# Seven block products for groups 2 to 4 of the last layer, and a shorter transposition of x^T between the layers

## The reference

```python
# 1: a recurrence over 768 time steps gives x, 3072 tokens of 320 channels
# 2: eight experts, x (3072 x 320), w1[e] (320 x 1024), w2[e] (1024 x 320)
for e in range(8):
    h = np.maximum(x @ w1[e], 0.0)
    out += P[:, e:e + 1] * (h @ w2[e])
# 3: the last layer, x = out, w_in (320 x 2048), w_out (2048 x 320)
h = x @ w_in
g = np.where(h > 0.0, h, np.exp(np.minimum(h, 0.0)) - 1.0)
return g @ w_out
```

## Time and profile before

| What | Value |
|---|---|
| Median of 3 runs | 2197.11 us (2195.76 to 2197.89) |
| Profiled execution, time | 2197.48 us |
| Profiled execution, span | 2195.5 us |
| TensorE matmul busy | 2166.0 us, 99% of the span |
| DVE busy | 1351.4 us, 62% |
| ScalarE busy | 809.8 us, 37% |
| GpSimd busy | 409.1 us, 19% |
| Experts' fast groups | about 667 to 1827 us |
| Last layer | 1827 to 2192 us |

### The profile page before, as it was taken

How to read it: one execution, slowest core, us unless ns; L and a number is a source line. 1 busy time by engine, 2 the same in 40 slices (tenths; PEclk the granted TensorE clock), 3 DMA queues, 4 the chain that set the end, 5 groups by cost and what they waited for, 6 DMA issues and landing times.

```text
span 2195.5 us, 35882 instructions
## 1 busy us (share of the span) xinstructions
PE 2166.0 (99%) x14692; PEld 1954.5 (89%) x14692; DVE 1351.4 (62%) x2429; ACT 809.8 (37%) x1429; POOL 409.1 (19%) x376
## 2 busy tenths in 40 slices
PE   8999999989999999999999999999999999999999
PEld 7899999878898999999999998999999998899898
DVE  6777777754457655555555555555555555666665
ACT  3433333323224333333333333333333333433333
POOL 4433333311143111111111111111111010010100
PEclk9999999999999999999999999999999999999999
DMA  6334333330101000000000000000000101000001
GB/s 102 64 59 64 65 61 60 60 91 29 47 20 46 27 1 27 27 1 27 27 1 27 27 1 27 27 1 27 27 1 27 27 1 27 1 27 27 1 16 58
DMA packets 193782, 70.51 MB, mean 32 GB/s; under 512 B 153424, under 2 KB 189776, under 8 KB 193616
## 3 DMA queue, kind: packets, MB, share of 16 engines
q1 hardware_dynamic: 193616, 68.19, 14.0%
HBM read 60.31 MB, written 7.86 MB: 31 GB/s over the span
## 4 chain that ended last, share of the span: by engine, by line
PE 97%; DVE 1%; ACT 0%; POOL 0%; issue 0%; DMA 0%; SPq 0%; ACTq 0%; DVEq 0%; POOLq 0%
PE up L1384 19%; PE up L1343 12%; PE yps L1441 9%; PE yps L1442 9%; PE yps L1443 9%; PE up L1391 7%; PE misc L1157 5%; PE yps L1360 4%; PE yps L1358 4%; PE yps L1359 4%; PE yps L1116 3%; PE up L1131 2%; PE up L1089 2%; PE up L1116 1%; PE up L1139 1%; PE misc L1150 1%
## 5 line engine op out<-in xcount | busy, mean ns | idle before, releaser
L1892 DVE SCALAR_TENSOR_TENSOR tok<-yps,prob,tok 128x320 f32<-128x320 f32 x672 | 343.1, 546 | 134.7 <-PE yps L1443 134.5
L1441 PE MATMUL yps<-w2h,hh 128*128 128x320 f32 x1344 | 414.9, 309 | 0.8 <-DVE hl L1875 0.3
L1443 PE MATMUL yps<-w2h,hl 128*128 128x320 f32 x1344 | 415.0, 309 | 0.0
L1442 PE MATMUL yps<-w2l,hh 128*128 128x320 f32 x1344 | 415.0, 309 | 0.0
L885 ACT ACTIVATE up<-up 128x512 f32<-128x512 f32 x252 | 146.7, 582 | 397.1 <-PE up L1384 395.5
L1441 PEld LDWEIGHTS yps<-w2h,hh 128*128 128x128 f32 x1344 | 252.5, 188 | 22.3 <-DVE hl L1875 2.0
L1442 PEld LDWEIGHTS yps<-w2l,hh 128*128 128x128 f32 x1344 | 252.3, 188 | 10.6
L1443 PEld LDWEIGHTS yps<-w2h,hl 128*128 128x128 f32 x1344 | 252.3, 188 | 0.0
L691 POOL TENSOR_TENSOR w1l<-w1l_raw,w1h 128x768 fp32r<-128x768 f32 x68 | 103.2, 1517 | 622.9 <-ACT w1h L796 622.9
L1875 DVE SCALAR_TENSOR_TENSOR hl<-up,hh 128x512 fp32r<-128x512 f32 x168 | 115.5, 688 | 161.3 <-ACT hh L897 161.3
L1875 DVE SCALAR_TENSOR_TENSOR hl<-hl_raw,hh 128x512 fp32r<-128x512 f32 x168 | 117.9, 702 | 147.8 <-ACT hh L897 147.8
(11 more groups left out here) (236 smaller groups left out, 4239.2 us busy)
## 6 DMA issues: line engine op xcount, KB each, us to landing
w2l_raw<-in_moe_w SPq DMA_DIRECT2D x16, 640.0 KB, 5.8
w1l_raw<-in_moe_w SPq DMA_DIRECT2D x32, 256.0 KB, 3.1
xr_raw<-x_dram SPq DMA_DIRECT2D x12, 512.0 KB, 4.0
w1l_raw<-in_moe_w SPq DMA_DIRECT2D x32, 128.0 KB, 3.9
wp<-in_w SPq DMA_DIRECT2D x24, 160.0 KB, 3.2
rp<-in_r SPq DMA_DIRECT2D x24, 160.0 KB, 3.1
vp<-in_v SPq DMA_DIRECT2D x48, 80.0 KB, 3.2
raw<-in_a SPq DMA_DIRECT2D x24, 160.0 KB, 3.7
```

Source lines behind the costliest of these rows:

```text
L1441: nc.tensor.matmul(o, hh[:, tile, c], wh, start=first, stop=False)
L1442: nc.tensor.matmul(o, hh[:, tile, c], wl, start=False, stop=False)
L1443: ins = nc.tensor.matmul(o, hl[:, tile, c], wh, start=False, stop=last)
L1892: nc.vector.scalar_tensor_tensor(out=acc, in0=yps[:, s, 0:DM], scalar=prob_of(blk * NSUB + s, e), in1=acc, op0=ALU.mult, op1=ALU.add).then ...
```

## The change

Groups 17 to 19 of the last layer are done in fast sets like the experts' (18 sets, numbered 84 to 101; the experts' are 0 to 83), with an order of their own (`second_set` on each engine). Group 16 stays plain. In a second set the odd block's down matmuls (`odd_down`) are issued within the next set, behind its fifth product; the next set's seventh and first product follow each other between the even block's two down slices. Each of the four tiles of a set goes through the exponential (`second_exp`), DVE's two operations (`elu`), the high part (`second_hi`) and the low part, which GpSimd makes (`second_lo`). Weights of the next group and the rest of the mixed tokens are made at places in the set called "first" and "middle" (`second_tasks`). The mixed tokens need raw rows of x^T, which ScalarE copies out of the transposes' bank (`raw_copy`). In group 16, ScalarE makes the mixed tokens of blocks 0 to 3 at steps 5 to 8, 12 to 14 and 18, and splits group 17's weights at the steps `WEIGHTS_AT`.

The tail rows of x^T are transposed once, into 64 rows; high and low part both come from these. Block 1 is transposed in the experts' last three sets as well, two tiles to a set. The output is stored by `s_facc` instead of `s_acc`. The exponentials and sums now lie where `hh` and `hl` will be written.

```diff
-    ALL_SETS = (G1 - FIRST_FAST) * SETS
+    EXPERT_SETS = (G1 - FIRST_FAST) * SETS
+    ALL_SETS = EXPERT_SETS + (G2 - 1) * SETS
+    PLAIN_STEPS = 3 * STEPS
...
+        exps, hh = twin("hh", [P, RING, TB])
         sums, hl = twin("hl", [P, RING, TB])
-        halves = xr.rearrange("p j t n -> p (j t) n")
-        ex, ge = halves[:, 0:2, :], halves[:, 2:4, :]
...
+        def raw_mixed(j):
+
+            return [spare[3], spare[4], spare[2], spare[1] if j == 2 else spare[5]]
+
+        def raw_rows(blk, t):
+
+            return mixed_a_raw[:, 2 * blk + t, :] if blk < 2 else spare[blk % 2 * 3 + t]
...
+        WEIGHTS_AT, TOKENS_AT = [9, 10, 11, 15, 16, 19], [12, 13, 14, 18]
...
-            return FIRST_FAST <= g < G1
+            return FIRST_FAST <= g and g != G1
+
+        def fast_no(g):
+            return g - FIRST_FAST if g < G1 else g - FIRST_FAST - 1
...
+        def second_tasks(g):
+
+            if g == G1 + 1:
+                return {(0, "middle"): ("weights", 0), (1, "first"): ("tokens", 0), (1, "middle"): ("tokens", 1),
+                        (2, "first"): ("tokens", 2), (2, "middle"): ("tokens", 3), (3, "first"): ("weights", 1),
+                        (3, "middle"): ("weights", 2), (4, "first"): ("weights", 3), (4, "middle"): ("weights", 4),
+                        (5, "first"): ("weights", 5)}
+            if g + 1 < GROUPS:
+                return {(1 + t // 2, ("first", "middle")[t % 2]): ("weights", t) for t in range(len(FAST))}
+            return {}
...
+        def tiles_within(i):
+
+            n = i - (EXPERT_SETS - 3)
+            return [(blk, t) for blk in range(2) for t in range(3)][2 * n:2 * n + 2] if n >= 0 else [None, None]
...
-                sp.wait_ge(s_acc, plain_no(GROUPS - 1) * NT + t + 1)
+                blk, sub = divmod(t, NSUB)
+                i = ALL_SETS - SETS + blk // 2 * FPAIRS + FPAIRS - 1
+                sp.wait_ge(s_facc, i * 2 * NSUB + blk % 2 * NSUB + sub + 1)
...
+            def mix_tokens(n):
+
+                j, second = n % TPAIRS, n >= TPAIRS
+                if second:
+                    pool.wait_ge(s_rawrows, 4 * (j + 1))
+                    pool.wait_ge(s_mixlo, 4 * n)
+                    pool.wait_ge(s_part, 6 * EXPERT_SETS)
...
+                t1, t2, t3, t4 = raw_mixed(j)
...
+                link(nc.gpsimd.tensor_tensor(t1, b12, b11, ALU.subtract))
+                link(nc.gpsimd.tensor_tensor(t2, b22, t1, ALU.subtract))
+                nc.gpsimd.tensor_tensor(t4, b21, t2, ALU.subtract).then_inc(s_mixsum, 1)
...
+            def second_lo(i, n, tile):
+
+                pool.wait_ge(s_fhi, 4 * i + n + 1)
+                nc.gpsimd.tensor_tensor(hl[:, tile, :], sums[:, tile, :], hh[:, tile, :].bitcast(F32), ALU.subtract)\
+                  .then_inc(s_flo, 1)
...
+            mix_tokens(3)
+            mixed_lo(3)
+            mix_weights(G1 + 1)
+            split_lo(G1 + 1, range(0, 3))
+            mix_tokens(4)
+            mixed_lo(4, range(0, 3))
+            split_lo(G1 + 1, range(3, 5))
+            mixed_lo(4, range(3, 4))
+            split_lo(G1 + 1, range(5, 6))
...
+                if g == G1 + 1 and n == 0:
+                    mix_tokens(5)
+                more("first")
+                second_lo(i, 0, 0)
+                if n == 0 and g + 1 < GROUPS:
+                    mix_weights(g + 1)
+                second_lo(i, 1, 1)
+                more("middle")
+                second_lo(i, 2, 3)
+                second_lo(i, 3, 2)
...
+            def raw_copy(blk, t):
+
+                if blk in (3, 5):
+                    act.wait_ge(s_mixlo, 4 * TPAIRS + 4 * (blk // 2 - 1) + 2)
+                if blk == 4:
+                    act.wait_ge(s_mixsum, TPAIRS + 2)
+                nc.scalar.activation(raw_rows(blk, t), x_bank(blk, t), ACT.Copy).then_inc(s_rawrows, 1)
...
+                    if t < 2:
+                        raw_copy(blk, t)
...
+                    if 5 <= k < 9:
+                        mixed_hi(3, k - 5)
+                    if k in WEIGHTS_AT:
+                        split_hi(G1 + 1, WEIGHTS_AT.index(k))
+                    if k in TOKENS_AT:
+                        mixed_hi(4, TOKENS_AT.index(k))
                     hi_second(n0 + k, k)
...
+            def second_exp(i, tile, src, ready, count):
+
+                act.wait_ge(ready, count)
+                act.wait_ge(s_fdown, i * 2 * NSUB - (NSUB if tile < 2 else 0))
+                nc.scalar.activation(exps[:, tile, :], src, ACT.Exp).then_inc(s_fexp, 1)
...
+            def second_set(i, more):
+
+                act.wait_ge(s_p1, i + 1)
+                act.wait_ge(s_add, 2 * i)
+                if i == EXPERT_SETS:
+                    act.wait_ge(s_lo, PLAIN_STEPS)
+                    act.wait_ge(s_down, PLAIN_STEPS * NSUB)
+                bank_copy(up[:, bank_b, :], up[:, bank_a, :])
+                act.wait_ge(s_part, 6 * i + 1)
+                bank_copy(up[:, bank_c, :], up[:, bank_b, :])
+                second_exp(i, 0, up[:, bank_a, :], s_part, 6 * i + 2)
+                more("first")
+                act.wait_ge(s_part, 6 * i + 4)
+                act.wait_ge(s_fge, 4 * (i - EXPERT_SETS) + 1)
+                bank_copy(up[:, bank_a, :], up[:, bank_b, :])
+                second_hi(i, 0, 0)
+                second_exp(i, 1, sums[:, 1, :], s_add, 2 * i + 1)
+                second_hi(i, 1, 1)
+                more("middle")
+                second_exp(i, 3, up[:, bank_a, :], s_part, 6 * i + 6)
+                second_exp(i, 2, sums[:, 2, :], s_add, 2 * i + 2)
+                second_hi(i, 2, 3)
+                if i + 1 < ALL_SETS:
+                    seventh_copy(i + 1)
+                second_hi(i, 3, 2)
...
                     else:
-                        nc.tensor.transpose(x_bank(blk, t)[0:TAIL, cols], tile[:, 2 * P:DM], ident[:])
-                        ins = nc.tensor.matmul(x_bank(blk, t)[TAIL:P, cols], tile[:, 2 * P:DM], ident[:],
-                                               start=True, stop=True)
...
                     pe.wait_ge(s_lo, FIRST_FAST * STEPS - 2)
-                wait(pe, s_flo, 4 * i)
+                elif i < EXPERT_SETS:
+                    pe.wait_ge(s_flo, 4 * i)
+                elif i == EXPERT_SETS:
+                    pe.wait_ge(s_lo, PLAIN_STEPS - 2)
+                else:
...
@@ -1460,24 +1654,19 @@
                 tail_terms(bank_c, buf, 2 * fp + 1, n0)
                 main_terms(bank_c, buf, fp, A22, t4, stop=True).then_inc(s_part, 1)
                 main_terms(bank_b, buf, fp, S1, t1).then_inc(s_part, 1)
-                pe.wait_ge(s_flo, 4 * i + 1)
-                fast_down(i, 0, 0, range(NSUB), first=True)
+                if i > EXPERT_SETS:
+                    odd_down(i - 1)
                 pe.wait_ge(s_copy, copies + 3)
                 tail_terms(bank_b, buf, 2 * fp + 1, n1).then_inc(s_part, 1)
                 tail_terms(bank_a, buf, 2 * fp, n1)
                 main_terms(bank_a, buf, fp, S4, b22, stop=True).then_inc(s_part, 1)
+                pe.wait_ge(s_flo, 4 * i + 1)
+                fast_down(i, 0, 0, range(NSUB), first=True)
+                if i + 1 < ALL_SETS:
+                    seventh_product(i + 1)
+                    first_product(i + 1)
                 pe.wait_ge(s_flo, 4 * i + 2)
                 fast_down(i, 0, 1, range(NSUB), last=True)
-                if i + 1 < ALL_SETS:
-                    seventh_product(i + 1)
-                if extra:
-                    extra()
-                pe.wait_ge(s_flo, 4 * i + 4)
-                for s in range(NSUB):
-                    if s == NSUB - 1 and i + 1 < ALL_SETS:
-                        first_product(i + 1)
-                    fast_down(i, 1, 1, [s], first=True)
-                    fast_down(i, 1, 0, [s], last=True)
...
             for k in (STEPS - 2, STEPS - 1):
-                down_product((plain_no(GROUPS - 1)) * STEPS + k, k, (GROUPS - 1) % 2)
+                down_product(FIRST_FAST * STEPS + k, k, G1 % 2)
+            seventh_product(EXPERT_SETS)
+            for i in range(EXPERT_SETS, ALL_SETS):
+                second_set(i)
...
+            def second_elu(i, n, tile, src):
+
+                dve.wait_ge(s_fexp, 4 * (i - EXPERT_SETS) + n + 1)
+                elu(tile, src).then_inc(s_fge, 1)
+
+            def add_second(i, tile, bank, ready):
+
+                dve.wait_ge(s_part, ready)
+                dve.wait_ge(s_copy, 1 + 4 * i)
+                dve.wait_ge(s_fdown, i * 2 * NSUB - (NSUB if tile == 1 else 0))
+                nc.vector.tensor_tensor(sums[:, tile, :], up[:, bank, :], seventh[:], ALU.add).then_inc(s_add, 1)
...
+            def second_set(i):
+
+                n = (i - EXPERT_SETS) % SETS
+                before = 2 * ((n - 1) % SETS // FPAIRS) + 1
+                if i == EXPERT_SETS:
+                    dve.wait_ge(s_down, PLAIN_STEPS * NSUB)
+                second_elu(i, 0, 0, up[:, bank_a, :])
+                add_second(i, 1, bank_c, 6 * i + 3)
```

(14 more changed lines are left out.)

262 lines of the change are left out of this document (167 added, 95 removed).

## The result

The changed kernel takes 2205.5 us (median of 7 runs, 2203.1 to 2206.3) where the kernel before takes 2196.9 us (7 runs, 2195.8 to 2197.9). The ratio is 1.0038, with a 95% interval of 1.0026 to 1.0049: 8.6 us slower. 2206 us was forecast, from a sum of +9.3 us. The profiled execution has a span of 2204.1 us, against 2195.5.

A forecast was written before the change was run, and what follows sets the result against it. TensorE was taken to bound the kernel, busy 2166.0 of 2195.5 us. Gains of 24.9 us against added stops and clock falls summed to +9.3 us on the profiled execution's 2197.5, less 0.4 to the median: 2206 us, range 2192 to 2214.

The forecast's parts named there:

- (b): Group 16's middle: TensorE stands still 3.7 us at step 13, 1.1 at step 10, 0.8 at the end: 5.6 us.
- (f): Smaller costs: DVE has two tiles in each of three experts' sets, 1.2 us in the last one (0 to 1.2).
- gain 1: Seven products in groups 17 to 19: 0.62 us saved per set, 11.2 us over 18 sets, other end 12.4.
- gain 2: x^T's tail transposed once: 2.0 us saved for each of 6 blocks, 12.0 us, other end 9.2.
- (a): Sets with a middle job: GpSimd holds DVE's third minimum, first product late in seven sets, 5.2 us; nothing if not held.
- (c): First new set, no odd block to fill it: bare chain, then first product 5.9 us late; together 8.5 us.
- (d): Group 18's first set: low part waits behind GpSimd's mixing of group 19's late-loaded weights; TensorE stands still 8.3 us.
- (e): The end: the last odd block has no set to hide in; TensorE waits 2.3 us for GpSimd's low parts.
- half clock: TensorE's clock falls behind the 5.9 and 8.3 us stops: 4.1 us less 1.0, so 3.1; ends 0 and 6.2.
- (1): Rival: TensorE's clock holds through the stops, 3.1 us less, 2203 us; chance 0.15.
- 2: Rival: GpSimd doesn't hold DVE's wide minima in the sets and group 16; change is faster, 2193 us; chance 0.16.
- the tight appointment: Rival: bank a's last read, 0.4 us ahead of the next first product, is missed in every set: +7 us, 2213; chance 0.22.

The follow-up runs named there:

- the experiment: The kernel before with only x^T's tail rows transposed once, block 1 left in group 16 and eight products kept: 2184.7 us, ratio 0.9946.
- experiments c: Changed kernel, but in the first new set GpSimd mixes group 18's weights behind its four low parts, and the middle job splits mixed tokens: 2200.3 us, ratio 1.0018.
- a: Changed kernel, but in every set GpSimd does its middle job behind the third low part instead of before it: 2197.6 us, ratio 1.0003 against the kernel before.
- e: Changed kernel, but the very last low part is done by DVE instead of GpSimd: 2203.2 us, ratio 1.0029 against the kernel before.
- experiment d: Changed kernel, but GpSimd mixes group 19's weights in group 18's second set, their splits one set later: 2194.3 us, ratio 0.9990 against the kernel before.
- b: Changed kernel, but in group 16 the tokens of blocks 2 and 3 are mixed before the third split of group 17's weights: 2201.3 us, ratio 1.0019.
- all edits: Changed kernel with three mixings moved, GpSimd's middle jobs behind the third low part, and the last low part on DVE: 2178.5 us, ratio 0.9915 against the kernel before.

## Why the prediction was right

The time was forecast within 1 us, and most stops came at the place, behind the instruction and in the number of sets that the layout on paper gave; the exceptions are one of the three of (b), which did not come, and (f), which has another cause. The sizes erred in both directions, and that the sum still fits is luck:

| term of the sum | forecast | after |
|---|---|---|
| gain 1, seven products | -11.2 (to -12.4) | -12.6 |
| gain 2, the tail | -12.0 (to -9.2) | -11.6 |
| gain 3, the wait of 1.7 us | -1.7 | -1.7 |
| (a) GpSimd's middle jobs | +5.2 | +3.4 |
| (b) group 16's middle | +5.6 | +3.3 |
| (c) first new set | +8.5 | +6.9 |
| (d) group 18's first set | +8.3 | +8.3 |
| (e) the end | +2.3 | +1.8 |
| (f) DVE's tiles in the last experts' set | +1.2 | +1.0, by GpSimd's mixing |
| half clock | +3.1 (0 to 6.2) | +7.0 |
| edges of stops | +0.1, within (b) | +2.9 |
| sum | +9.3 | +8.7 |

*Gain 1.* The end of the range was the right value: a set that nothing disturbs is shorter than the mean of the experts' 71 intervals. The first and the last of ScalarE's seven copies of the seventh product from group 18's fifth set on:

```profile
2097.34 0.60 ACT L974 ACTIVATE seventh<-up 128x512 f32<-128x512 f32 x1
...
2179.54 0.60 ACT L974 ACTIVATE seventh<-up 128x512 f32<-128x512 f32 x1
```

Six intervals are 82.20 us, 13.70 each, 0.72 less than four steps of 3.605 us; 18 of these would be 13.0. *Gain 2* and *gain 3* hold. The tail's transposes show at 1822.76 us and the stop (f) behind them (0.60 us for the four besides the stop, as in the experiment; the other five blocks take 0.35):

```profile
1822.76 0.60 PE L1434 MATMUL misc<-ident,tok 128*64 128x128 f32 x4
1824.40 0.38 PE L1590 MATMUL yps<-w2h,hh 128*128 128x320 f32 x1 [1.04 <-DVE tok L2090]
```

*(d)* is exact, and moving the mixing takes the whole stop away (2194.3 us without it). *(a)*: exactly seven sets stop, and only those with a job in the middle; the holding is shown by the minimum of 1.40 against 0.43 us. It was over-priced by half; which part of the layout made it so was not tested. *(b)*: the stop at step 13 is 3.04 instead of 3.7 us, the one at step 10 is 0.27 instead of 1.1 and none is seen at the end, so most of the error lies in the two small ones. *(c)*: the late first product is 4.92 instead of 5.9 us, and 3.6 us of it went with the wait for the mixed weights. *(e)* is within 0.5 us. *(f)* is within 0.2 us in size, but for the wrong reason: DVE's second tile is done in time, and what holds DVE there is GpSimd's mixing of the tokens of blocks 0 and 1, which the prediction put at nothing in this set. All stops: 31.1 us forecast, 24.7 found.

*The clock* is the term that was mis-sized the most. The step that failed is "Both long stops [...] are emptier than that stretch was, so I count two falls": the two falls came and cost 3.7 us, but shorter stops, 3.04 and 1.78 us, made it fall as well, 3.2 us more (a third fall in (b) was the other end of the range, the one at the end was not foreseen), and the 1.0 us taken off for waits that a slower TensorE doesn't meet was not seen. The edges of the stops, 0.2 to 0.3 us each, were not in the sum at all but for one 0.1. With stops 6.4 us too dear, what follows stops 6.7 us too cheap and gains 1.0 us too small, the sum came out right by luck: these errors cancelled.

The rivals: the clock did not hold (1), which only the trace tells, since 2203 us lies within the interval of the time; the wide minimum is held, so 2 is out; and the tight appointment is kept in every set of group 19 (3), which has no stop at all.

Left open: what decides whether the clock falls behind the stops of 3.0 and 1.8 us (below). Gain 1 was not run by itself; its size is read from the traces.

## What to carry to other kernels

When a change takes work off the engine that sets the time, lay the other engines' queues out beside the shortened step, and look for an instruction that waits for a load or a slower engine with something urgent queued behind it: four such orders, and one low part on the slower engine at the end, cost this change 27 us, and moving each by a few places, the last one to DVE, turned 0.4% slower into 0.85% faster. Price a stop of a pipelined matmul engine at more than its length in the list of waits: here 0.2 to 0.3 us for its edges, and 1.5 to 2.2 us where the clock falls behind it. Work handed from DVE to GpSimd is not free even when GpSimd is idle for three quarters of the time: what counts is which DVE instruction is due while GpSimd works.

## What the runs showed of the hardware

The stops of 3.5 us and more had TensorE's clock at its lower level behind them in all ten cases in six profiles. The stop of 3.0 us in group 16 had it in four profiles (the changed kernel and experiments c, a and e) and not in that of experiment d, at the same length and with the same work around it. The stop of 1.8 us at the end had it in three profiles (the changed kernel, c and b) and not in two (d and a). No stop of 1.33 us or less was followed by a fall, nor was the one of 1.71 us in the two profiles that have it (the kernel before, and the one with the tail alone). Times agree: the eleven runs of experiment d lie between 2192.0 us (mean granted clock 0.996) and 2197.9 us (0.994), the five with all edits, whose trace has no fall behind 1780 us, within 1.4 us. So what a stop of 1.8 to 3 us costs differs from one execution to the next, and one profile doesn't price it. The Trainium skill ("TensorE: Matmul & The Clock Gate", What's actually happening) says that the chip watches TensorE's activity on a beat of its own, which the kernel doesn't start; the two outcomes of one and the same stop agree with that, but no run here shows the beat.

Four transposes of 64 columns cost the same as four of 128. TensorE's timeline of the changed kernel, the tail of block 0:

```profile
1800.70 0.60 PE L1434 MATMUL misc<-ident,tok 128*64 128x128 f32 x4
1801.05 0.48 PE L1535 MATMUL up<-xt,w1h 128*128 128x512 f32 x1
1801.37 0.39 PE L1535 MATMUL up<-xt,w1l 128*128 128x512 f32 x1
```

0.35 us for the four, as for the full-width ones of the earlier trace rows, and 0.32 us instead of 0.23 for the matmul behind them.

How long DVE is held is set by where GpSimd's instruction ends. From 667 us on, in the trace of the changed kernel, 31 of DVE's minima of 512 columns are longer than 0.5 us (0.61 to 1.96, alone 0.43): each of them ends 0.28 or 0.29 us behind the GpSimd instruction beside it. Of DVE's 512-column operations with both operands in SBUF, 12 are longer than 0.79 us (0.80 to 1.75, alone 0.69): each ends 0.55 us behind GpSimd's.
